# Opening rows issued from GpSimd's queue and the first half's MLP weights issued from ScalarE's queue, in a fused mLSTM, MLP and expert kernel

## What is computed

```python
# 1: a gated linear recurrence per head, computed in chunks of 128 steps
m_new = max(f + m, i);  f_s = exp(f + m - m_new);  i_s = exp(i - m_new)
C = f_s * C + i_s * outer(v, k);  n = f_s * n + i_s * k
y = sigmoid(o) * (C @ q) / max(abs(n @ q), 1)
# 2: the two-layer part, 320 -> 2048 -> 320
x = leaky_relu(x @ w_in, 0.01) @ w_out
# 3: eight dense experts, 320 -> 1024 -> 320, summed with weights P
P = exp(x @ w_gate - max), eight rounds of row and column normalising
out = sum_e P[:, e] * (relu(x @ w1[e]) @ w2[e])
```

## Time and profile before

| | |
|---|---|
| median of 3 runs | 933.89 us (933.8 to 934.96) |
| the profiled execution | 933.91 us, its span 932.2 us |
| PE busy | 925.9 us (99% of the span) |
| DVE, POOL, ACT busy | 635.1, 424.8, 354.2 us |
| chain that ended last | PE 97%, DVE 2%, ACT 1% |
| PE clock granted | 1.0 in all slices (2.4 GHz) |

### The profile page before, as it was taken

The page is one execution under the profiler, slowest core; times in us unless marked ns, Lnnn a source line. Parts: engine busy times, 40 slices in busy tenths (PEclk is TensorE's granted clock), DMA queues, the critical chain, the costliest instruction groups (busy, mean ns, idle before and its releaser), DMA issues.

```text
span 932.2 us, 16714 instructions
## 1 busy us (share of the span) xinstructions
PE 925.9 (99%) x6508; PEld 888.5 (95%) x6518; DVE 635.1 (68%) x1064; ACT 354.2 (38%) x671; POOL 424.8 (46%) x483
## 2 busy tenths in 40 slices
PE   8999999999999999999999999999999999999998
PEld 6999888888899999999999999999999999999998
DVE  6887444466778899867666676666766666666665
ACT  6674443354443332333333332333243233323221
POOL 4562311074586554667543751754375166336000
PEclk9999999999999999999999999999999999999999
DMA  7990221012021112021201211110121111110000
GB/s 125 200 164 10 86 65 34 1 35 54 20 67 29 29 35 69 1 69 35 68 3 34 69 36 35 34 56 14 34 60 44 36 35 38 32 34 1 30 29 29
DMA packets 83084, 43.77 MB, mean 47 GB/s; under 512 B 54366, under 2 KB 82398, under 8 KB 83006
## 3 DMA queue, kind: packets, MB, share of 16 engines
q1 hardware_dynamic: 82830, 42.61, 17.9%
q10 hardware_dynamic: 176, 0.10, 0.0%
HBM read 39.13 MB, written 2.11 MB: 44 GB/s over the span
## 4 chain that ended last, share of the span: by engine, by line
PE 97%; DVE 2%; ACT 1%; DMA 0%; issue 0%; ACTq 0%; DVEq 0%
PE psB L1738 12%; PE psB L1740 12%; PE psB L1739 12%; PE psA L1651 9%; PE psA L1724 9%; PE psA L1723 9%; PE psA L1722 9%; PE psA L1721 9%; PE psB L1671 2%; PE psB L1670 2%; PE psB L1672 2%; PE psB L1554 2%; PE psA L1531 2%; PE psB L1677 1%; PE psB L1676 1%; PE psA L1706 1%
## 5 line engine op out<-in xcount | busy, mean ns | idle before, releaser
L713 POOL TENSOR_TENSOR wst<-raw_w,wst 128x128 fp32r<-128x128 f32 (+2 forms) x192 | 162.0, 856 | 300.8 <-ACT wst L933 173.6
L1738 PE MATMUL psB<-w2s,gh 128*128 128x320 f32 x768 | 238.6, 311 | 0.0
L1740 PE MATMUL psB<-w2s,gl 128*128 128x320 f32 x768 | 237.3, 309 | 0.0
L1739 PE MATMUL psB<-w2s,gh 128*128 128x320 f32 x768 | 237.3, 309 | 0.0
L1047 ACT ACTIVATE gh<-part 128x512 fp32r<-128x512 f32 x192 | 110.9, 625 | 243.7 <-DVE part L1435 243.6
L1441 DVE SCALAR_TENSOR_TENSOR gl<-part,gh 128x512 fp32r<-128x512 f32 x192 | 158.0, 863 | 63.0 <-ACT gh L1047 62.5
L1724 PE MATMUL psA<-xop,wst 96*128 96x256 f32 x672 | 190.2, 283 | 0.0
L1723 PE MATMUL psA<-xop,wst 128*128 128x256 f32 x672 | 190.2, 283 | 0.0
L1722 PE MATMUL psA<-xop,wst 128*128 128x256 f32 x672 | 190.2, 283 | 0.0
L1721 PE MATMUL psA<-xop,wst 128*128 128x256 f32 x672 | 190.0, 283 | 0.0
L1738 PEld LDWEIGHTS psB<-w2s,gh 128*128 128x128 f32 x768 | 144.6, 188 | 0.3 <-issue 0.2
(11 more groups left out here) (202 smaller groups left out, 1361.0 us busy)
## 6 DMA issues: line engine op xcount, KB each, us to landing
raw_w<-in_moe_w_dram SPq DMA_DIRECT2D x32, 320.0 KB, 3.2
raw_w<-in_moe_w_dram SPq DMA_DIRECT2D x32, 256.0 KB, 2.6
raw_w<-in_moe_w_dram SPq DMA_DIRECT2D x96, 64.0 KB, 2.5
qs<-in_q_dram SPq DMA_DIRECT2D x12, 160.0 KB, 3.3
ks<-in_k_dram SPq DMA_DIRECT2D x12, 160.0 KB, 4.0
og<-in_o_gate_dram SPq DMA_DIRECT2D x12, 160.0 KB, 3.6
vz<-in_v_dram SPq DMA_DIRECT2D x12, 160.0 KB, 4.0
out_dram<-acc SPq DMA_DIRECT2D x5, 320.0 KB, 2.3
```

Of the source, the lines that this page charges most:

```text
L713: return pool.tensor_tensor(dst, raw, high.bitcast(F32), ALU.subtract)
L1738: pe.matmul(bank, gh[:, slot, cols], w2[:, f, 0, :], start=first, stop=False)
L1739: pe.matmul(bank, gh[:, slot, cols], w2[:, f, 1, :], start=False, stop=False)
L1740: last = pe.matmul(bank, gl[:, slot, cols], w2[:, f, 0, :], start=False, stop=end)
```

## The change

There are four edits, all in the recurrence's opening and in who issues the weights' loads.

1. The five row DMAs of chunk 0 for `rhs` (batch 0: k = 0, 1; batch 1: k = 0, 1, 2) and the bounce move to POOL, ahead of its first `corner`. Each row has a semaphore of its own there. SP keeps the two for `lhs` and the one for `rhs` k = 2 of batch 0. SP's order becomes rows of batch 0, q and k of unit 2, `lhs` of batch 1, v of units 0 and 1, q and k of unit 3.
2. The loads of the first half's weights move from SP to ACT: the first two behind `exponentials(0, 0)`, the others behind `out_gate` of units 4, 5 and 6.
3. `warm(9)` becomes `warm(6)`, and `warm(6)` becomes `warm(4)`.
4. PE's `intra(0, 0)` is no longer split around `transposes(0, 2)`: the transposes come first, then both halves.

```diff
@@ sync
             load_gates_out(0, range(B))
-            load_qk(2)
             sp.wait_ge(lhs_ok, 1)
             sp.wait_ge(copied_ok, 2)
             sp.wait_ge(parts0_ok, 1)
-            first_rows(sp, 0, (-1, PARTS - 1))
+            first_left(0)
+            sp.dma_start(rhs[0][AR + PARTS - 1:AR + PARTS, 0, :, :], parts0[0:H, 1, PARTS - 1, :]).then_inc(row0_in[0], 16)
+            load_qk(2)
+            first_left(1)
             load_v(0)
-            first_rows(sp, 1, (-1, *range(PARTS)))
-            sp.wait_ge(parts_ok, 1)
-            sp.dma_start(parts_d.rearrange("b h c s k t -> (b h c) s k t"), parts[:]).then_inc(bounced, 16)
             load_v(1)
...
-            first_w1(0)
-            first_w2(0)
@@ gpsimd
             pool.wait_ge(blank, 1)
+            pool.wait_ge(copied_ok, 2)
+            pool.wait_ge(parts0_ok, 1)
+            for b, k in ((0, 0), (0, 1), (1, 0), (1, 1), (1, 2)):
+                pool.dma_start(rhs[0][AR + k:AR + k + 1, b, :, :],
+                               parts0[b * H:(b + 1) * H, 1, k, :]).then_inc(row0_sw[b][k], 16)
+            pool.wait_ge(parts_ok, 1)
+            pool.dma_start(parts_d.rearrange("b h c s k t -> (b h c) s k t"), parts[:]).then_inc(bounced, 16)
             corner(0)
@@ scalar
             qk_copies(0, 0)
-            act.wait_ge(lhs_ok, 1)
-            act.wait_ge(parts0_ok, 1)
-            act.wait_ge(copied_ok, 2)
-            first_rows(act, 0, range(PARTS - 1))
             qk_copies(0, 1)
...
             exponentials(0, 0)
+            first_w1(0)
+            first_w2(0)
             exponentials(0, 1)
...
                 out_gate(n)
+                if n == U_IT:
+                    first_w1(1)
+                if n == U_IT + 1:
+                    first_w2(1)
+                if n == U_IT + 2:
+                    first_w1(KT)
@@ tensor, exponents
-                    pe.wait_ge(row0_in[b], ROWS0)
+                    pe.wait_ge(row0_in[b], 16 * (2 - b))
+                    for k in range(2 + b):
+                        pe.wait_ge(row0_sw[b][k], 16)
@@ tensor, opening
-            warm(9)
+            warm(6)
...
-            warm(6)
+            warm(4)
...
-            intra(0, 0, (0,))
             transposes(0, 2)
-            intra(0, 0, (1,))
+            intra(0, 0)
```

More of the change, by code:

```diff
@@ L243, in build @@
         row0_in = [sem(f"row0_in{b}") for b in range(B)]
+        row0_sw = [[sem(f"row0_sw{b}{k}") for k in range(2 + b)] for b in range(B)]
         rows_in = [[sem(f"rows_in{s}{b}") for b in range(B)] for s in range(2)]
-        ROWS0, ROWS = (PARTS + 1) * 16, 2 * 16
+        ROWS = 2 * 16
         blank = sem("blank")
@@ L403, in out_gone @@
             return o_used, (before - 2) * BP + (NTB - 1) * PP + p + 1
[L405 to L412, removed]
         def chunk_rows(eng, c, b):
@@ L463, in _, with first_left @@
             sp.dma_start(gf[:], f_gate.rearrange("b h s -> (b h) s")).then_inc(gates_in, 16)
+            def first_left(b):
+                sp.dma_start(lhs[0][0:AR, b, :], parts0[b * H:(b + 1) * H, 0, :, :]).then_inc(row0_in[b], 16)
             def load_qk(n):
@@ L509, in load_pair @@
                 sp.dma_start(raw_w2[q][:], w2[e, cols, :].rearrange("(f p) d -> p f d", p=P)).then_inc(raw_in[q], 16)
[L511 to L522, removed]
             load_qk(0)
@@ L562, in _ @@
                     chunk_rows(sp, (n + B) // B, n % B)
[L563 to L568, removed]
             for a in range(KT):
@@ L797, in _, with first_w1, first_w2 @@
         def _(act):
+            def first_w1(k):
+                if k < KT:
+                    act.dma_start(raw1[:, k, :], w_in[k * P:(k + 1) * P, 0:FW]).then_inc(w1_in[k], 16)
+                else:
+                    act.dma_start(raw1[0:DR, KT, :], w_in[KT * P:DM, 0:FW]).then_inc(w1_in[KT], 16)
+                    act.dma_start(raw1[DR:P, KT, :], w_in[KT * P:DM, 0:FW]).then_inc(w1_in[KT], 16)
+            def first_w2(half):
+                rows = slice(half * NF // 2, (half + 1) * NF // 2)
+                act.dma_start(raw2[:, rows, :], w_out[0:FW, :].rearrange("(f p) d -> p f d", p=P)[:, rows, :]).then_inc(w2_in[half], 16)
             def out_gate(n):
```

## The result

The changed kernel took 939.39 us (median of 6 runs, 937.53 to 940.61), the kernel before beside it 933.85 us (933.71 to 934.96). The ratio is 1.0053, with a 95% interval from 1.0042 to 1.0063: slower by 5.5 us, outside the forecast range (932.3 to 936.6 us). The profiled execution took 939.54 us, its span 937.8 us; before, 932.2 us. So the span is 5.6 us longer.

What follows compares the result with a forecast made beforehand. PE, busy 925.9 of 932.2 us, was taken to bound the kernel. The span, 932.2 - 0.3 + 0.3 + 0.1 = 932.3 us, plus 1.71 us around it gave 934.0 us; range 932.3 to 936.6 us.

Steps and rivals of the forecast that it cites:

- the term for the weight loads: Early weight loads on ACT fill the DMA engines; bounced rows land up to 1 us late, taken as +0.3 us.
- The term for v of unit 0: SP issues this load at 12.3 instead of 10.54 us; it lands 3.2 us later, at 15.5 us.
- (a): ACT loses two row issues, 1.86 us; unit 1's copies, row weights and scores can come up to 1.9 us earlier.
- (b): Five filler matmuls cut from PE's opening, 1.2 us; they turn into a wait for rows, worth nothing.
- (c): SP loses three rows and the bounce; unit 2's exponents, waiting for its last piece, start at 19.1 instead of 19.43 us: -0.3 us.
- The price of POOL's issues: Each DMA issue on POOL in the opening was taken to cost 0.9 us, bounded by 0.44 and 1.86 us.
- rival 1: POOL's issues are dear or held until DVE ends at 12.01 us: +3.2 us, 937.1 us; chance 0.20.
- The corner cut: POOL's `corner(0)`, behind its new DMA issues, was to start at 14.3 us against 14.21 before: a tie.
- the +0.1 us: `first_w1(1)`, issued behind the gate of unit 4, might land late for ACT and delay PE's transposes: +0.1 us.
- Rival 2: Weights late or in the way, both prices at their ends: 1.7 us more, 935.6 us; chance 0.12.

Runs made afterwards that it cites:

- experiment 1: Changed kernel with all the first half's weight loads back on SP at their old places: 933.38 us, ratio 0.9998.
- experiment 5: Changed kernel with SP issuing the pieces of bounced rows for units 2 and 3 ahead of q and k of unit 3: 938.74 us, ratio 1.0046.
- experiment 8: Changed kernel with 12 filler matmuls on PE ahead of the exponents of unit 2: 941.13 us, ratio 1.0069.
- experiment 9: Changed kernel with 9 filler matmuls ahead of the product with v of unit 0 and 9 ahead of the exponents of unit 2: 937.41 us, ratio 1.0031.
- experiment 7: Changed kernel with the first two weight loads on ACT behind the second exponential instead of the first: 939.23 us, ratio 1.0047.
- experiment 10: Changed kernel, weight loads back on SP, unit 2's pieces of bounced rows held until PE's product with v of unit 0: 937.37 us, ratio 1.0031.
- experiment 11: Changed kernel with weight loads back on SP and the five filler matmuls put back (9 and 6): 933.70 us, ratio 0.9991.
- experiment 4: Changed kernel with all weight loads on SP, the first two between v of unit 0 and v of unit 1: 940.91 us, ratio 1.0068.
- experiment 2: Kernel before with only the first half's weight loads moved to ACT as in the change: 938.93 us, ratio 1.0056.
- experiment 6: Changed kernel with only w_in (0.5 MB) early on ACT, w_out ahead of the exponential of unit 3: 938.62 us, ratio 1.0043.
- experiment 3: Changed kernel with the first two weight loads still on ACT, but ahead of the exponential of unit 3: 933.61 us, ratio 0.9995.

## Why the prediction was wrong

**The step that failed** is the term for the weight loads in the sum: "The bounced rows may land up to 1 us late. I take a third of that, +0.3 us". The view it rests on was read rightly: the loads bring over 5 us of engine time, and the engines do fill up (0.98 from 15 to 20 us). The conclusion was not drawn. If over 5 us of engine time go in ahead of what PE waits for, some of PE's data is late by a good part of them. The runs put 3.05 us there (exponents of unit 2 at 22.48 instead of 19.43 us), three times the end that I had called the worst, and 3.64 us against experiment 1, where the gain of the opening edits is taken out. The term for v of unit 0 had the same fault: I let it land "3.2 us later", its duration in a window with a DMA share near 0.5, and it took 5.2 us; in experiments 5, 8 and 9, with the same loads, PE could start on it 6.35, 6.02 and 6.30 us after its issue. The loads also left 1 us earlier than I had them.

**A cost was left out of the sum**: the loads of SP behind the megabyte are not only slow to land, their issue stalls (3.51 us for one that took 0.88 us before and 0.63 in experiment 1). The sum had SP free to issue the pieces at 16.0 us; they went at 18.53 us. Experiments 5 and 7 show that this is one channel of two, and that removing it alone helps little. It could have been read in the trace of before: there SP issued the same two loads at 25.30 and 25.98 us, and its next 6 KB piece, 0.69 us at 16.48 us, took 3.02 us:

```profile
28.59 3.02 SPq L417 DMA_DIRECT2D lhs<-parts_d  x1
```

**And a second one**: what a wait of PE does to its clock. I priced each wait at its own length. The clock added 2.57 us to 3.05 us of lateness (experiments 9 and 10). 3.05 + 2.57 = 5.62 us, the loss in the trace. No row of before shows it, since PE, once started, never waited more than 0.61 us there (of the 55 runs of the kernel before that stand beside the experiments, four had a mean clock of 0.998 and took 935.31 to 935.47 us, so it is not quite free of it); the term "with both ends" should have had an upper end for it.

**Point by point.** (a) ACT's `qt` of unit 1 came at 9.63 us, not 8.9: PE's transposes of unit 0 took 0.85 and 0.70 us instead of 0.49 each in that trace, and the second started 0.7 us later; the cause is open. In experiment 1 it stood at 8.88 us, as forecast. (b) The filler as worth nothing: PE waited 0.33 us for the rows in experiment 1, so some 0.9 us of 1.2 were free for use, and how much reached the end stays open (experiment 11). (c) The last wait before, ahead of the exponents of unit 2, was read rightly as the landing of the piece, and so was the record missing from that row: 22.30 - 19.43 = 2.87 us is what experiment 9 measured for the same stretch. The price of POOL's issues was too high, 0.57 us against 0.9; ACT's 0.93 was the wrong neighbour. It made rival 1 the strongest slow case at 0.20, and no run shows POOL's issues held while DVE works: the five went out in 2.85 us, between 9.44 and 12.29 us, while DVE computed the second set of parts. The corner cut came at 14.07 us (forecast 14.3), and that is luck: POOL's issues were out at 12.84 us, the cut followed ACT's exponential, and so its time does not settle the price of an issue as the forecast had it. `first_w1(1)` was issued at 42.06 us, landed in 4.2 us, and its cast at 47.66 us followed without a wait: the +0.1 us was not needed. Rival 2 named the right place, without the stalled issue and the clock, and gave it at most 935.6 us (its two ends add 1.6 us to the forecast, not 1.7). Rival 1's 937.1 us leaves out the 0.4 us of the weights' terms.

**One queue or two.** The Trainium skill, page "DMA: Bandwidth & Descriptors", section "Issuing engines are not separate DMA queues", says that DMAs of all issuing engines run on the same 16 DMA engines and interleave, so that a second issuing engine saves issue time alone. The traces agree: weights on ACT's queue made SP's v of units 0 and 1 land in 5.2 and 8.4 us instead of 3.6 and 4.0 (experiment 1), and experiment 4, all on SP, was no better. By that sentence the second queue of edit 2 could not have kept the weights out of the way; the prediction used the rows of the same fact and priced them too low.

## What to carry to other kernels

Before a large load is moved to an earlier spot, list what is issued shortly before and after it and who waits for that; its whole engine time is my estimate of the upper end of the delay, whatever queue it is on (here 5.4 us; the longest wait for the pieces was 4.13 us, and v of unit 1 landed in 8.5 instead of 3.2 us, both in experiment 2; with 0.5 MB, 2.4 us by the same rate, the loads of v, q and k took 2.1 to 2.7 us longer in experiment 6 than in experiment 1), and a stalled issue holds back what stands behind it as well. Price a wait of the bounding engine at more than its length where its clock can fall: the trace of before, without such a wait, can't show it, so the upper end takes in a stretch of work at the other clock level. The same loads on the same queue, 10 us later, cost nothing that can be told.

## What the runs showed of the hardware

- A DMA issue is no fixed price: the 160 KB load of k of unit 3 took SP 0.63, 0.88 and 1.25 us to issue (experiment 1, before, experiment 3) and 3.51, 3.65, 3.68 and 4.64 us with 0.5 to 1.15 MB of weights just issued (the changed kernel, experiments 6, 4 and 2), and everything behind it on SP waited. The DMA share does not tell the two apart: from 14 to 16 us it was 1.04 in experiment 1 and 0.93 in the changed kernel.
- A load of 6 KB took 4.9 us to land beside the megabyte (experiment 7), 2.2 us without (before).
- Five 2 KB row issues took POOL 0.57 us each and the 144 KB bounce 0.54 us; such rows had taken ACT 0.93 us each. They went out without a gap while DVE worked.
- A DMA issue that stands behind an exponential in ACT's stream does not wait for its end: the first left at 12.99 us, with the exponential running from 12.98 to 14.00 us (the changed kernel), and at 15.41 us, the exponential's own start, in experiment 7.
- PE's granted clock stood at 1.2 GHz instead of 2.4 behind PE's idle times of 2.00 us (experiment 10), 2.19 us (the changed kernel) and 2.21 us (experiment 7), while PE worked without a gap, and came back later; behind the 0.61 us of before it had stayed at 2.4. It need not fall during the wait: in experiment 5 the wait ended at 18.74 us, the slice from 18 to 20 us stands at 1.00 and the one from 20 to 22 us at 0.61. Where filler took the place of the idle time it never fell (experiment 9).
- In the changed kernel a lower mean clock of a run went with a longer time: 937.53 us at 0.998, 938.52 to 939.54 at 0.996, and 940.28 to 940.61 at 0.995.
